# Batch 1 of a gated linear attention: exponents from shifted rows in DRAM, decays by transfer, products on 64-row tiles

## The reference

```
m_new = max(f + m, i);  f_stab = exp(f + m - m_new);  i_stab = exp(i - m_new)
C = f_stab * C + i_stab * v k^T;   n = f_stab * n + i_stab * k
y = sigmoid(o) * (C q) / max(|n q|, 1)
```

## Time and profile before

| | |
|---|---|
| median of 3 runs | 289.72 us (288.74 to 290.57) |
| the profiled execution | 291.4 us, of which the traced span is 289.3 us |
| PE busy | 264.7 us, 91% of the span |
| PEld, DVE, ACT, POOL busy | 247.3, 180.0, 115.4, 85.7 us |
| DMA | 26289 packets, 25.68 MB |
| chain that ended last | PE 74%, DVE 7%, issue 7%, POOL 5%, ACT 4% |

### The profile page before, as it was taken

How to read it: one execution, slowest core, us unless ns; L and a number is a source line. 1 busy time by engine, 2 the same in 40 slices (tenths; PEclk the granted TensorE clock), 3 DMA queues, 4 the chain that set the end, 5 groups by cost and what they waited for, 6 DMA issues and landing times.

```text
span 289.3 us, 5204 instructions
## 1 busy us (share of the span) xinstructions
PE 264.7 (91%) x1964; PEld 247.3 (85%) x1964; DVE 180.0 (62%) x401; ACT 115.4 (40%) x212; POOL 85.7 (30%) x102
## 2 busy tenths in 40 slices
PE   0598788999999999999999999999999999999675
PEld 0587677679799999999999997899999999999564
DVE  7988877486878568535866303537653168742991
ACT  2664545488444432443432223322232332232731
POOL 4415578903654553155004000000040000130710
PEclk9999999999999999999999999999999999999988
DMA  7699987664765143220000010000000100000101
GB/s 219 155 274 321 302 265 219 212 198 124 208 189 132 57 142 91 84 68 3 0 0 2 3 66 2 0 0 2 0 2 23 45 1 2 0 2 0 56 13 68
DMA packets 26289, 25.68 MB, mean 89 GB/s; under 512 B 13977, under 2 KB 22009, under 8 KB 26265
## 3 DMA queue, kind: packets, MB, share of 16 engines
q1 hardware_dynamic: 21976, 18.72, 22.2%
q10 hardware_dynamic: 4288, 6.64, 7.1%
HBM read 23.34 MB, written 2.02 MB: 88 GB/s over the span
## 4 chain that ended last, share of the span: by engine, by line
PE 74%; DVE 7%; issue 7%; POOL 5%; ACT 4%; DMA 1%; SPq 0%; ACTq 0%; POOLq 0%; DVEq 0%
PE shared L1172 30%; PE h_ps L1306 22%; PE s_ps L1210 4%; PE hv_ps L1191 2%; PE s_ps L1244 2%; PE hv_ps L1195 2%; DVE gate L1039 2%; PE shared L1271 2%; PE h_ps L1244 2%; POOL qs L597 2%; PE shared L1221 1%; DMA mask_sb<-mask 1%; PE shared L1318 1%; DVE prob L930 1%; PE shared L1256 1%
## 5 line engine op out<-in xcount | busy, mean ns | idle before, releaser
L1104 DVE SCALAR_TENSOR_TENSOR h_lo<-shared,h_hi 128x384 fp32r<-128x384 f32 x48 | 26.5, 557 | 40.2 <-ACT h_hi L824 40.1
L1306 PE MATMUL h_ps<-ch_hi,h_hi 128*128 128x320 f32 x144 | 45.4, 315 | 0.0
L1306 PE MATMUL h_ps<-ch_hi,h_lo 128*128 128x320 f32 x144 | 44.5, 309 | 0.0
L824 ACT ACTIVATE h_hi<-shared 128x384 fp32r<-128x384 f32 x48 | 23.1, 488 | 53.2 <-PE shared L1172 50.1
L1306 PE MATMUL h_ps<-ch_lo,h_hi 128*128 128x320 f32 x144 | 44.3, 308 | 0.0
L1172 PE MATMUL shared<-u_hi,ch_hi 128*128 128x384 f32 x96 | 33.1, 344 | 0.1
L1172 PE MATMUL shared<-u_lo,ch_hi 128*128 128x384 f32 x96 | 32.6, 339 | 0.0
L1172 PE MATMUL shared<-u_hi,ch_lo 128*128 128x384 f32 x96 | 32.5, 339 | 0.0
L1210 PE MATMUL s_ps<-q_in,k_in 128*128 128x128 f32 x192 | 27.1, 300 | 3.9 <-DMA q_in<-qT 3.9
L1210 PEld LDWEIGHTS s_ps<-q_in,k_in 128*128 128x128 f32 x192 | 25.2, 211 | 6.1 <-DMA q_in<-qT 4.5
L1039 DVE SCALAR_TENSOR_TENSOR gate<-x,conv_sb,gate 128x384 f32<-128x384 f32 x44 | 29.0, 668 | 1.0
(11 more groups left out here) (181 smaller groups left out, 550.3 us busy)
## 6 DMA issues: line engine op xcount, KB each, us to landing
G_all<-G_scratch SPq DMA_DIRECT2D x11, 512.0 KB, 5.8
o_sig<-on ACTq DMA_DIRECT2D x2, 960.0 KB, 6.7
k_in<-kT SPq DMA_DIRECT2D x24, 80.0 KB
q_in<-qT SPq DMA_DIRECT2D x24, 80.0 KB
kn_in<-kn SPq DMA_DIRECT2D x12, 160.0 KB, 4.3
v_in<-vn SPq DMA_DIRECT2D x12, 160.0 KB, 4.8
stage<-ch ACTq DMA_DIRECT2D x3, 640.0 KB, 4.3
out<-o_sb SPq DMA_DIRECT2D x12, 160.0 KB, 1.8
```

Source lines behind the costliest of these rows:

```text
L824: act.activation(h_hi[i % 3][:], ps_of(key)[:, 0:T], ACT.Relu).then_inc(hi_ready, 1)
L1104: took(dve.scalar_tensor_tensor(out=h_lo[i % 3][:], in0=ps_of(key)[:, 0:T], scalar=0.0, in1=h_hi[i % 3][:].bitcast(F32), op0=ALU.max, op1= ...
L1306: last = pe.matmul(h2_ps[t][:, 0:DM], a[:, tile_cols(t)], w[:, f, :], start=(f == 0 and n == 0), stop=(f == FT - 1 and n == 2))
```

## The change

1. **k_in and the state lose their zeros.** A score product is `k_in[64g : 64g+40]` against the same rows of `q_in`, a matmul on a tile of 64 rows; the two groups alternate. The state products do the same from `state`, which is double-buffered and written once; `apart` is gone. `delta` goes through the heads with the groups in turns.
2. **PE's order in a step** is now: state products of u-1, scores of u, value products of u-1 (the last two were in the other order, with the state products among the value products), token products, delta. DVE waits for both groups of scores before it multiplies the first.
3. **Batch 1 gets its exponents masked by transfer.** G of batch 1 is saved with each head's 128 values followed by 127 of -1e30 (`G_wide`). `skew(u)` copies, DRAM to DRAM, 128 rows x 8 heads x 128 values (1024 pieces of 512 bytes), row p starting p values later in the source and in the target, so that `Z_dram` holds for partition p the values of G with -1e30 where the key position is past the query; the first head's triangle comes from `fill_masked`, six copies of the 64 KB mask. `masked_chunk(u)` then loads 512 KB into `G_all`. DVE's `exponents` are gone for batch 1: ACT does exp(G + A) with A as a per-partition bias, eight instructions of 128x128.
4. **Batch 1 gets its decays by transfer.** ACT takes exp of all of G once (16x768), SP saves it to DRAM, and `decay_chunk(u)` copies a chunk's row to the partitions (two transfers of 128 KB) for POOL. ACT's `decays` are gone for batch 1.
5. **Places.** `fill_masked` is issued after chunk 4; the first two `skew`s and the save of exp(G) after chunk 5, between a wait for `Z_filled` and a wait for `E_saved`; only then does SP issue chunk 6, in the order k, q, kn, v, masked G. `exps(6)` moves in ACT's program to just ahead of the `o_sig` load and `hidden_a(0)`. Two memsets of `k_in` go, and the first loads wait for two memsets instead of four.

```diff
-        k_in = [sb("k_in0", [P, 2, HG * L]), sb("k_in1", [P, 2, HG * L], at=a_at + 4 * S)]
+        k_in = [sb(f"k_in{k}", [P, HG * L]) for k in range(2)]
...
-        state = sb("state", [ROWS, HG * D1])
-        apart = [sb(f"apart{k}", [P, 2, HG * D1]) for k in range(2)]
+        state = [sb(f"state{k}", [ROWS, HG * D1]) for k in range(2)]
...
-        G_dram = nc.dram_tensor("G_scratch", [NU, H * L], F32, kind="Internal").ap()
+        G_dram = nc.dram_tensor("G_scratch", [NC, H * L], F32, kind="Internal").ap()
+        G_wide = nc.dram_tensor("G_wide", [NC, H, 2 * L], F32, kind="Internal").ap()
+        E_dram = nc.dram_tensor("E_scratch", [NC, H * L], F32, kind="Internal").ap()
+        Z_ROW = (H + 1) * L
+        Z_dram = nc.dram_tensor("Z_scratch", [NC, P, Z_ROW], F32, kind="Internal").ap()
...
+            dst = G_wide[:, :, 0:L].rearrange("c h l -> h c l") if b else \
+                G_dram.rearrange("c (h l) -> h c l", l=L)
...
+            def fill_masked():
+                for c in range(NC):
+                    sp.dma_start(Z_dram[c, :, 0:L], mask).then_inc(Z_filled, 16)
+            def skew(u):
+                c = u - NC
+                src = bass.AP(tensor=G_wide.tensor, offset=c * H * 2 * L, ap=[[1, P], [2 * L, H], [1, L]])
+                dst = bass.AP(tensor=Z_dram.tensor, offset=c * P * Z_ROW, ap=[[Z_ROW + 1, P], [L, H], [1, L]])
+                sp.dma_start(dst, src).then_inc(Z_made[u % 2], 16)
+            def masked_chunk(u):
+                k, c = u % 2, u - NC
+                if c >= 2:
+                    sp.wait_ge(exp_ready, 2 * (u - 1))
+                else:
+                    sp.wait_ge(expo_ready, 2 * (u - 1))
+                    sp.wait_ge(decay_ready, u - 2)
+                sp.wait_ge(Z_made[k], 16 * (c // 2 + 1))
+                sp.dma_start(G_all[k][:], Z_dram[c, :, 0:H * L]).then_inc(G_in[k], 16)
+            def decay_chunk(u):
+                k, c = u % 2, u - NC
+                if c >= 3:
+                    sp.wait_ge(qs_ready, with_state(u - 2))
+                    sp.wait_ge(kept_ready, with_both(u - 2))
+                for g in range(2):
+                    sp.dma_start(decay_in[k][64 * g:64 * g + 64, :],
+                                 E_dram[c:c + 1, g * HG * L:(g + 1) * HG * L].broadcast_to([64, HG * L])
+                                 ).then_inc(decay_loaded[k], 16)
             def k_chunk(u):
-                users = k_users(u)
-                if len(users) > 1:
-                    sp.wait_ge(s_ready, 2 * (users[-2] + 1))
+                if u >= 2:
+                    sp.wait_ge(s_ready, 2 * (u - 1))
                 for g in range(2):
-                    sp.dma_start(k_in[k_buffer(u)][64 * g:64 * g + D, g, :],
-                                 kT[u, g]).then_inc(k_loaded[k_buffer(u)], 16)
+                    sp.dma_start(k_in[u % 2][64 * g:64 * g + D, :], kT[u, g]).then_inc(k_loaded[u % 2], 16)
...
             def chunk(u):
-                G_chunk(u)
+                if u < NC:
+                    G_chunk(u)
                 k_chunk(u)
                 q_chunk(u)
-                kn_chunk(u)
+                if u % NC < NC - 1:
+                    kn_chunk(u)
                 v_chunk(u)
+                if u >= NC:
+                    masked_chunk(u)
+                    if u > NC:
+                        decay_chunk(u)
+                    if u + 2 < NU:
+                        skew(u + 2)
...
-            sp.wait_ge(zeroed, 4)
             k_chunk(0)
+            sp.wait_ge(zeroed, 2)
...
+            fill_wide()
...
+                if u == 4:
+                    fill_masked()
                 if u == 5:
                     sp.dma_start(conv_sb[:], conv).then_inc(conv_in, 16)
+                    sp.wait_ge(wide_filled, 16)
+                    sp.wait_ge(Z_filled, 16 * NC)
+                    skew(NC)
+                    skew(NC + 1)
+                    sp.wait_ge(E_made, 1)
+                    sp.dma_start(E_dram.rearrange("c (h l) -> h c l", l=L),
+                                 E_row[H:2 * H, :].rearrange("h (c l) -> h c l", l=L)).then_inc(E_saved, 16)
+                    sp.wait_ge(E_saved, 16)
...
+                    if b:
+                        pool.wait_ge(decay_loaded[k], 32 * ((n + 1) // 2))
+                    else:
+                        pool.wait_ge(decay_ready, with_state(u))
...
             def exps(u):
+                if u >= NC:
+                    act.wait_ge(G_in[u % 2], 16 * (u // 2 + 1))
+                    act.wait_ge(hv_ready, u - 1)
+                    for g in range(2):
+                        for j in range(HG):
+                            h = g * HG + j
+                            col = (u - NC) * B * H + H + h
+                            last = act.activation(prob[(2 * u + g) % 4][:, tile_cols(j)], G_all[u % 2][:, tile_cols(h)],
+                                                  ACT.Exp, bias=A_col[:, col:col + 1])
+                        last.then_inc(exp_ready, 1)
+                    return
...
+                    act.wait_ge(G_ready, 2)
+                    act.activation(E_row[:], G_row[:], ACT.Exp).then_inc(E_made, 1)
+                if b == 0 and n + 1 < NC:
...
+            exps(NC)
             act.wait_ge(y_ready, NC - 1)
             act.wait_ge(y_last, 1)
             act.dma_start(o_sig[:], on[1].rearrange("(c p) d -> p c d", p=P)).then_inc(o_in, 16)
...
-                        if q == 0 and d == 1:
-                            exps(NC)
                     if q == 0:
                         piece(act, 4)
                         output_gate(1)
-                        decays(NC + 1)
...
-                    new = apart[(u + 1) % 2]
-                    grown(new[0:64, 0, :], slice(0, 64))
-                    last = grown(new[64:ROWS, 1, :], slice(64, ROWS)).then_inc(apart_ready, 1)
-                    if n < NC - 2:
-                        last = grown(state[:], slice(0, ROWS))
-                        took(last, key)
-                    else:
-                        dve.wait_ge(apart_ready, with_next(u))
-                        dve.sem_inc(shared_done[J[key] % 2], 1)
+                    took(grown(state[(u + 1) % 2][:], slice(0, ROWS)), key)
...
-                if n + 1 < NC:
+                if b == 0 and n + 1 < NC:
                     exponents(u + 1)
...
-            exponents(NC, (0,))
...
+                v = u - 1
+                if n >= 1 and v >= 1:
+                    pe.wait_ge(ht_ready, v)
+                if n >= 2:
+                    pe.wait_ge(qs_ready, with_state(v))
+                    done(pe, ("delta", v - 1))
+                    for j in range(HG):
+                        for g in range(2):
+                            r = slice(64 * g, 64 * g + D)
+                            pe.matmul(hv_ps[64 * g:64 * g + D1, tile_cols(j)], state[v % 2][r, j * D1:(j + 1) * D1],
+                                      qs[v % 2][r, tile_cols(j)], start=(j == 0), stop=False)
+                if n < NC:
+                    pe.wait_ge(q_loaded[k], 32 * (u // 2 + 1))
+                    pe.wait_ge(k_loaded[k], 32 * (u // 2 + 1))
+                    if u >= 1:
+                        pe.wait_ge(prob_ready, 2 * u)
+                    for j in range(HG):
+                        for g in range(2):
+                            r = slice(64 * g, 64 * g + D)
+                            last = pe.matmul(s_ps[g][:, tile_cols(j)], k_in[k][r, tile_cols(j)],
+                                             q_in[k][r, tile_cols(j)], start=True, stop=True)
+                            if j == HG - 1:
+                                last.then_inc(s_ready, 1)
                 if n >= 1:
-                    v = u - 1
                     pe.wait_ge(prob_ready, 2 * v + 2)
                     pe.wait_ge(v_loaded[v % 3], 16 * (v // 3 + 1))
-                    if v >= 1:
-                        pe.wait_ge(ht_ready, v)
-                    if n >= 2:
-                        pe.wait_ge(qs_ready, with_state(v))
-                        pe.wait_ge(apart_ready, with_next(v - 1))
                     for j in range(HG):
-                        if n >= 2:
-                            for g in range(2):
-                                pe.matmul(hv_ps[64 * g:64 * g + D1, tile_cols(j)],
-                                          apart[v % 2][:, g, j * D1:(j + 1) * D1], qs[v % 2][:, tile_cols(j)],
-                                          start=True, stop=False)
                         for g in range(2):
                             last = pe.matmul(hv_ps[64 * g:64 * g + D1, tile_cols(j)], v_in[v % 3][:, g * HG + j, :],
-                                             prob[(2 * v + g) % 4][:, tile_cols(j)], start=(n < 2), stop=True)
+                                             prob[(2 * v + g) % 4][:, tile_cols(j)],
+                                             start=(n < 2 and j == 0), stop=(j == HG - 1))
                     last.then_inc(hv_ready, 1)
```

(30 more changed lines are left out.)

49 lines of the change are left out of this document (27 added, 22 removed).

## The result

The changed kernel takes 306.14 us (median of 4 runs, 303.89 to 306.85), beside 289.47 us for the kernel before: a ratio of 1.0575, 95% interval 1.0522 to 1.0627. The forecast was 294.4 us with a range of 283 to 300. The profiled execution took 306.85 us, its span is 304.9 us, 15.6 us more than before. Some executions are a few per cent slower than the others of the same kernel: in what follows medians count them, ratios leave them out, and two of the traces (exponentials behind the weights, transposes behind the channel products) are of such an execution.

The account below looks back on a forecast made before the run. Batch 0's attention was taken as bound by transfers, batch 1's by PE. Terms + 6.0 (late a_hi) + 0.8 (clock) - 2.4 (scores) + 1.2 (order) - 0.9 (DVE, ACT) = + 4.7 us gave 294.4 us, range 283 to 300.

Parts of the forecast that it names:

- I take 38 ns, halfway: Assumed price of each 512-byte mask or skew piece in SP's queue, between 28 ns by bytes and 47 ns average.
- the transfers at the end of batch 0: Masked G(6) lands late behind mask copies, skews and exp(G)'s save, so a_hi comes at 62.7 us, 6.0 us later.
- My own bound at a doubled price: If each DRAM to DRAM packet costs twice 47 ns, a_hi comes at 73.7 us, 17.0 us late.
- hidden at a share of 0.72: Batch 1's added skews and decays raise the DMA share from 0.41 to about 0.72, which keeps transfers hidden.
- about the same: ACT exchanges two exponentials and two decays for eight biased exponentials of 2.4 us, with about equal work.
- Loads go one after the other: Weight loads of the score row tiles do not overlap, 98 ns each: 0.41 us gained a chunk, 2.4 us in all.
- the rival: Row tiles load beside each other, scores gain 1.04 us a chunk; chance 0.28 if a_hi is late, 0.17 in time.
- The order in a step: With scores moved, only delta hides ACT's ht copy before turn_y: 1.2 us lost, between 0.5 and 2.
- Clock: PE stands some 5 us before a_hi, then runs at half clock: 0 to 1.6 us lost, 0.8 taken.
- DVE and ACT: DVE loses eight exponentials a chunk and two state copies; PE's two waits on them, 0.45 and 0.40 us, gain 0.9.
- the second, late with overlapping tiles: a_hi late by 6.0 us but row tiles load in parallel: - 0.8 us, 288.9 us, chance 0.28.
- my own fastest case: Masked G(6) in time, a_hi 0.2 us late, and row tiles overlap: - 7.4 us, 282.3 us, chance 0.17.

Follow-up runs that it names:

- exponentials behind the weights: Changed kernel with chunk 6's exponentials moved in ScalarE's program from ahead of hidden_a(0) to behind the second output gate: 308.85 us, ratio 1.0658 to the kernel before.
- transposes behind the channel products: Row tiles with batch 1's G, exponents and decays as before, later v loads, and batch 1's turn_y behind the channel products: 297.88 us, ratio 1.0244.
- straight writes: Changed kernel with skewed write's target rows aligned, in three versions (both sides straight, 4096-byte pieces, target only): 295.02, 295.44, 295.91 us, once each; batch 1's values differ.
- the destination alone was straight: Changed kernel whose skewed write starts each row at its own DRAM row, reads still shifted; batch 1's values differ: 295.91 us, once.
- the early store: Changed kernel with the store of exp(G) issued by ScalarE right behind its exp, not by SP behind the skewed writes: 305.40 us, once.
- late values: Row tiles with batch 1's G, exponents and decays as before, and v from chunk 7 loaded only after the previous chunk's scores are taken: 293.10 us, ratio 1.0166.
- the matmul half alone: Only 64-row tiles, single state and PE's new order; G, exponents and decays of batch 1 as in the kernel before: 293.94 us, ratio 1.0149.
- GpSimd behind the exponents: Row tiles with batch 1's G, exponents and decays as before; GpSimd weighs v from chunk 7 only after that chunk's exponents: 288.83 us, ratio 0.9974.
- the early exponents: Row tiles, batch 1's decays by transfer, no masked rows, GpSimd waiting for exponents, and chunk 7's exponents ahead of h_lo(0): 290.20 us, ratio 1.0040.

## Why the prediction was wrong

**The step that failed** is the price of a piece, "I take 38 ns, halfway", in the transfers at the end of batch 0. While the shifted pieces pass, the queue's mean packet costs 89 to 104 ns; with straight writes it costs 27 to 34. I had priced them by the mean packet of a queue that holds no such write. The mechanism was right in each link: exp(G) behind the skews, SP standing for it, chunk 6 behind that, then masked G(6), the exponentials, and `a_hi` last, at 70.16 us and not at 62.7. Of these 7.5 us, 3.5 are the landing of exp(G) (56.5, not 53.0), 1.0 the issues behind it (3.3 us, not 2.2), and 3.0 the landing of masked G(6) (8.02 us, not 5.0); the exponentials took 2.4, as said. Where the destination alone was straight, `a_hi` came at 62.98 us and the time was 295.91, beside my 62.7 and 294.4. So with a price near the assumed one the sum comes out, though not term by term, and there by luck: exp(G) landed at 50.6 (not 53.0), and masked G(6) took 6.8 us (not 5.0). My own bound at a doubled price said 73.7; it stood in the text and was left out of the range.

**A second term was missing.** I let the transfers end in front of `a_hi` and called those of batch 1 hidden at a share of 0.72. But the skews of chunks 8 to 11 (issued at 60.17, 70.11, 88.89 and 99.78 us) pass with the weights of the first channel pass, at a share of 1.05 in 61 to 76 us, 0.84 in 76 to 89 and 1.09 in 89 to 99.5. On the way to chunk 7's state products PE's two stands grew from 0.45 and 0.40 us to 1.60 and 3.80. ScalarE's longer exponentials ahead of `h_hi`, which I had called "about the same", are 1.1 us of that, and the rest is the weights, whose loads took 7.27 and 5.20 us. The half clock adds some 1.2 (below), and two cheaper groups of scores take off 1.7: near the + 4.2 us measured. With straight writes this way was + 0.6, + 0.8 and + 3.1 us instead of + 4.2 (once each). The late exponentials and the early store show how strong it is: each took away what held `a_hi` and left the time where it was or worse. In a settled step the share was 0.47 and they are hidden, as I said.

**Row tiles.** "Loads go one after the other" was wrong. A step's PE part, which answers to the earlier trace rows:

```profile
113.23 1.07 PE L1259 MATMUL hv_ps<-qs,state 40*41 40x128 f32 x16
114.23 1.16 PE L1270 MATMUL s_ps<-q_in,k_in 40*128 40x128 f32 x16
115.33 1.08 PE L1280 MATMUL hv_ps<-prob,v_in 128*41 128x128 f32 x16
116.23 0.61 PE L1296 MATMUL shared<-wv,kn_in 128*64 128x41 f32 x16
117.19 0.55 PE L1306 MATMUL shared<-ident_r,ht 105*128 105x105 f32 x4 [0.35 <-ACT ht L794]
```

(Start, duration, [idle before].) Scores take 1.10 us (114.23 to 115.33), not 1.98, a gain of 0.88 where I took 0.41 and the rival 1.04. State and value products take 1.00 + 0.90, as the 1.88 of before: 0, as forecast. Delta's 16 take 0.96 with the wait in it, 0.61 without, so 0.08 of the possible 0.35 is gained. By the Trainium skill ("TensorE: Matmul & The Clock Gate", LDWEIGHTS) 128 columns load in 107 ns; here 16 such loads on alternating row tiles pass in 1.10 us, 69 ns each, so the trace does not agree if the rule is taken for the spacing of loads into tiles of different rows. The spacing bears out the Trainium skill's "TensorEngine Tiling (Array Packing)", Key Properties, that different tiles load and multiply in parallel.

**The order in a step.** Forecast 1.2 us in all for the ht waits, measured 1.8 in four waits, 0.35 in a settled step where I had 0.1. With the scores' gain and delta's (0.88 + 0.08 - 0.35) that makes the step 0.6 us shorter (10.53 to 9.91), but up to `a_hi`, where transfers set the pace, the row tiles brought nothing: `a_hi` stood at 55.3 to 58.8 us, 56.8 in the mean, in the eight kernels that have them without the masked rows, beside 56.65.

**Clock.** I took 0.8 us. It fell to half for 61.6 to 75.3 us and again for 95.8 to 99.2, both behind a stand of PE. The second stretch can be priced: nine products of the same form take 2.55 us from 96.45 and 1.31 from 100.49, so 1.2 us. The first lies in the + 0.9 us between `a_hi` and channels 1, so both together cost some 2 us, an estimate from these rows.

**DVE and ACT.** DVE 24 us less busy, as said, and worth nothing where I had put its gain (0.9 us), since PE stood 1.60 and 3.80 us for `h_lo` in those places, behind later weights.

Of my cases the second, late with overlapping tiles, has both mechanisms, and no case had the size. My range of 283 to 300 also leaves out the 282.3 of my own fastest case.

## What to carry to other kernels

Before a layout in DRAM is used to save engine work, time its write alone with its real addresses: a shift of 4 bytes a row about tripled its price here. Count a new transfer against everything that still has to pass the same engines behind it, not only against who waits for it first. And before an engine's load is moved earlier, look at what ran undisturbed because it was late.

## What the runs showed of the hardware

- While DRAM to DRAM pieces of 512 bytes pass whose written address shifts by 4 bytes a row, a packet costs 89 to 104 ns in the mean of the queue, and 27 to 34 ns when only the read address shifts. Pieces of 4096 bytes were no faster in the end (295.44 and 295.02 us, once each).
- A VectorE instruction with two SBUF inputs that is issued beside a GpSimd instruction ended, in most cases, 0.14 to 0.15 us behind that one: it took 0.84 us beside `wv` and 1.63 beside `ch_lo`, instead of 0.34. The one beside `kept` ended only behind two further GpSimd instructions (3.25 us with late values, 3.26 in the matmul half alone); why this one did not get its turn stays open. With the mask in PSUM eight took 2.15 us beside `ch_lo`. The Trainium skill ("SBUF — State Buffer", SBUF: two separate sides) describes this as an exclusive lock on a port pair that VectorE and GpSimd share, held for the whole instruction; the trace agrees, but for the case of `kept`.
- PE's mean granted clock in 18 to 40 us was 1.00 before (busy for 19.07 of 22 us) and between 0.69 and 1.00 in the eight kernels with row tiles and without masked rows: 0.69 with GpSimd behind the exponents (busy for 19.70 us), 1.00 with the early exponents (18.11). What brings the half clock there stays open; it cost nothing visible, since `a_hi` came at 57.26 and 58.80 in these two.
